# Hash products of a head in four column groups, masks placed by way of a DRAM scratch, high parts in three transfers

## The chip, the core and the metric

The kernel runs on one core of a Trainium2 chip. The metric is the device time of an execution in microseconds, less is better. The engines are named as in the profile: PE (TensorE's products), PEld (its weight loads), DVE (VectorE), ACT (ScalarE), POOL (GpSimd) and SP (SyncE, which here only issues transfers). SPq is SP's queue of issues.

## The reference

Three stages in a row. The change lies in the first.

```
# stage 1: attention within hash buckets; 2 x 8 heads, 768 tokens, head_dim 64, proj (64, 6)
q_bucket = sum(((q @ proj) > 0) * 2**bit);  k_bucket likewise
scores = where(q_bucket == k_bucket, (q @ k.T) / 8, -1e9)
x = softmax(scores) @ v
# stage 2: MLP 512 -> 2048 -> 512 with g = P(h) / Q(h), h = x @ w_in
# stage 3: mixture of 8 experts, each token to the one of its largest gate logit
```

## The kernel before

Head m = 2 i + par has pair i and parity par; most tiles exist twice, one for each parity. A head is worked in six steps c of 128 queries, each against all 768 keys. Every engine runs its own written-out order (`step(i, c)`), a loop over the pairs, and semaphores tie the engines together.

A head's q and k (64 + 64 columns) are loaded side by side (`load_qk`), transposed by PE in two halves into the bank ps_p (`turn_qk`, L459) and copied by ACT to qkT, 128 rows of 768 tokens: q in rows 0 to 63, k in rows 64 to 127 (`copy_qk`, L790). POOL makes the high parts qkT_hi (L1347) and the low parts. SP carries the high parts to their places by four SBUF to SBUF transfers (`place_hi`, L291): to k_mask, q_mask, k_cross and q_cross.

The hash bits come from `hash_qk` (L466): hash_w, 128 x 64, times the two halves of qkT. The first half of the tokens goes to rows 0 to 63 of ps_p, the second to rows 64 to 127. Each group of 64 rows holds 12 rows for q from its row 0 on and 12 for k from its row 32 on. DVE compares them with thresholds in one operation over 128 x 384 (`mask_rows`, L1014), into mask_st, and SP carries 12 rows at a time to rows 64 to 75 of q_mask and k_mask (`place_masks`, L297, four transfers a head). A score product over those 76 rows then holds the dot product and a large negative number where the buckets differ (L481); a second product adds the low parts (L483).

ps_p is shared: `turn_qk` of the next head waits for `masked`, and `hash_qk` for the copies. Within PE's step order, `turn_qk` first half stands at the start of a head, its second half in step 3, `hash_qk` at the end of step 4, and the first score product of the next head in step 4 too. That product waits for `mask_in` and `hi_in`. DVE's `mask_rows` stands at the end of step 5, behind the copy of turned probabilities (L1045).

SP's order for head m: masks of head m+1; the row inverses of head m-1 to a DRAM scratch (L309); v of head m+1 (L282); the inverses back as scale_row (L314), behind a wait for their landing; a piece of w_in (L285); q and k of head m+4, behind PE's second half of transposes (L278, L279); x of head m-2 to xT (L305); the high parts of head m+2. All waits there are on one line, L261 (`hold`). Four heads have less: the first has no masks or inverses to move in the loop, and the last four no q and k to load.

The first head does without transfers: ACT copies its high parts (L832) and DVE writes its masks straight from ps_p (`mask_first`, L1004).

Of the kernel before, what the change touches and what calls it, by code (L numbers as in the profile page):

```python
# [16 lines left out]
ALU = mybir.AluOpType  # L17
ACT = mybir.ActivationFunctionType
AX = mybir.AxisListType
F32 = mybir.dt.float32  # L20
# [3 lines left out]
P = 128  # L24

def fused_kernel(nc, q, k, v, proj, w_in, w_out, mlp_a, mlp_b, w_gate, w_ogate, w1, w2, out):
# [25 lines left out]
    ZK = 32  # L53
    HC = 64
    PAD = 8
    assert MAX_SLOTS % 2 == 1 and FE == 2 * 512 and 2 * D == P and S % (2 * P) == 0 and CD * 2 == NH and GN == HALF and KR <= P and MR <= ZK

    inv_dram = nc.dram_tensor("row_inverse_scratch", (2, S), F32).ap()
    x2_dram = nc.dram_tensor("mlp_out_scratch", (TOK, DM), F32).ap()

    with ExitStack() as ctx:
# [22 lines left out]
        with ExitStack() as stage_ab:  # L84
# [4 lines left out]
            with ExitStack() as stage_a:  # L89
                sb = sbuf(stage_a)  # L90
                q_mask = [sb(f"q_mask{i}", [P, S], F32R) for i in range(2)]
                k_mask = [sb(f"k_mask{i}", [P, S], F32R) for i in range(2)]
                q_cross = [sb(f"q_cross{i}", [P, S], F32R) for i in range(2)]
# [4 lines left out]
                k_cross = [sb(f"k_cross{i}", [P, S], F32R) for i in range(2)]  # L98
                v_raw = [sb(f"v_raw{i}", [P, QT, D]) for i in range(2)]
# [8 lines left out]
                hash_w = sb("hash_w", [P, HC])  # L108
                hash_thr = sb("hash_thr", [P, 4])
                iota_p = sb("iota_p", [P, 1])  # L110
# [20 lines left out]
        with ExitStack() as stage_c:  # L131
# [64 lines left out]

        (ident_made, iota_made, zero_made, consts_in, ab_in, hash_made, coef_ps, coef_made, abs_made) = map(sem, (
            "ident_made", "iota_made", "zero_made", "consts_in", "ab_in", "hash_made", "coef_ps", "coef_made", "abs_made"))
        qk_in = [sem(f"qk_in{i}") for i in range(2)]
# [73 lines left out]
        def _(sp):  # L273
# [25 lines left out]

# [27 lines left out]
            place_hi(1)  # L327
            sp.wait_ge(masked, 2)
            place_masks(1)
            load_v(1, 1)  # L330
# [117 lines left out]
        def _(pe):  # L448
# [13 lines left out]
            def hash_qk(i, par):  # L462

                pe.wait_ge(qk_copied, 4 * i + 2 * par + 2)
                for hb in range(2):
                    mm = pe.matmul(ps_p[HC * hb:HC * (hb + 1), 0:HALF], hash_w[:],  # L466
                                   qkT[:, hb * HALF:(hb + 1) * HALF], start=True, stop=True)
                mm.then_inc(hashed, 1)

            def scores(i, c, first=False):  # L470

                par, j, slot = c // QT, c % QT, c % 2
                if j == 0:
                    pe.wait_ge(mask_in[par], 64 * (i + 1))
                    pe.wait_ge(hi_in[par], 64 * (i + 1))
                    pe.wait_ge(qk_parts, 4 * i + 2 * par + 2)
# [76 lines left out]
            keep_clock(2)  # L553
            pe.wait_ge(hash_made, 6)
            hash_qk(0, 0)
# [3 lines left out]
            pe.wait_ge(zero_made, 3)  # L559
# [4 lines left out]
            scores(0, 1, first=True)  # L564
            pe.wait_ge(masked, 1)
            hash_qk(0, 1)
# [211 lines left out]
        def _(act):  # L778
# [51 lines left out]
            for target, rows, part in ((k_mask, slice(0, D), slice(D, P)), (k_cross, slice(0, D), slice(D, P)),  # L830
                                       (q_mask, slice(0, D), slice(0, D)), (q_cross, slice(D, P), slice(0, D))):
                act.activation(target[0][rows, :], qkT_hi[part, :], ACT.Copy).then_inc(hi_in[0], 16)  # L832
            act.wait_ge(qk_parts, 2)
# [157 lines left out]
        def _(dve):  # L991
# [5 lines left out]
            def mask_first():  # L997

                dve.wait_ge(hashed, 1)
                for hb in range(2):  # L1000
                    cols = slice(hb * HALF, (hb + 1) * HALF)
                    for target, row in ((k_mask, HC * hb + ZK), (q_mask, HC * hb)):
                        rows = slice(row, row + MR)
                        dve.tensor_scalar(target[0][D:KR, cols], ps_p[rows, 0:HALF], hash_thr[rows, 2:3],  # L1004
                                          hash_thr[rows, 3:4], ALU.is_ge, ALU.mult).then_inc(mask_in[0], 16)
                dve.wait_ge(mask_in[0], 64)
# [41 lines left out]
            def step(i, c):  # L1048
# [8 lines left out]
                if c % QT == 5 and there(i + 1, 0):  # L1057
# [6 lines left out]
            dve.memset(hash_w[:], 0.0).then_inc(zero_made, 1)  # L1064
            dve.memset(hash_thr[:], 0.0).then_inc(zero_made, 1)
            dve.wait_ge(zero_made, 3)
            dve.wait_ge(iota_made, 1)
            dve.tensor_scalar(hash_thr[:, 0:1], iota_p[:], float(BITS), TINY, ALU.is_lt, ALU.mult).then_inc(abs_made, 1)
            dve.tensor_scalar(hash_thr[:, 1:2], iota_p[:], float(ZK + BITS), TINY,
                              ALU.is_ge, ALU.mult).then_inc(abs_made, 1)  # L1070
            dve.wait_ge(abs_made, 2)
            dve.tensor_tensor(hash_thr[0:HC, 2:3], hash_thr[0:HC, 0:1], hash_thr[0:HC, 1:2],
                              ALU.add).then_inc(hash_made, 1)
            for hb in range(2):
                dve.memset(hash_thr[HC * hb:HC * hb + ZK, 3:4], 1.0).then_inc(abs_made, 1)
                dve.memset(hash_thr[HC * hb + ZK:HC * (hb + 1), 3:4], -BIG).then_inc(abs_made, 1)
            dve.wait_ge(hash_made, 1)
            dve.tensor_copy(hash_thr[HC:P, 2:3], hash_thr[0:HC, 2:3]).then_inc(hash_made, 1)
            dve.wait_ge(consts_in, 32)
            dve.tensor_copy(hash_w[0:D, 0:BITS], proj2[0:D, :]).then_inc(hash_made, 1)  # L1080
            dve.tensor_scalar(hash_w[0:D, BITS:MR], proj2[0:D, :], -1.0, None, ALU.mult).then_inc(hash_made, 1)
            dve.tensor_scalar(hash_w[D:P, ZK:ZK + BITS], proj2[D:P, :], -1.0, None, ALU.mult).then_inc(hash_made, 1)
            dve.tensor_copy(hash_w[D:P, ZK + BITS:ZK + MR], proj2[D:P, :]).then_inc(hash_made, 1)
            dve.wait_ge(abs_made, 6)
            dve.wait_ge(hash_made, 6)
            hi_of_first()
# [254 lines left out]
        def _(pool):  # L1341
            def hi_of_qk(i, par):

                pool.wait_ge(qk_copied, 4 * i + 2 * par + 2)
                if 2 * i + par > 0:
                    pool.wait_ge(hi_in[1 - par], 64 * (i + par))
                pool.tensor_scalar(qkT_hi[:], qkT[:], 1.0, 0.0, ALU.mult, ALU.add).then_inc(qk_hi_made, 1)  # L1347
# [207 lines left out]
```

## Time and profile before

| | |
|---|---|
| median of 3 runs | 822.98 us (821.36 to 823.01) |
| the profiled execution | 822.91 us |
| its span, first to last instruction | 820.9 us |
| PE busy | 785.3 us (96%) |
| DVE, ACT, POOL busy | 81%, 72%, 42% |
| granted clock of TensorE, mean | 0.986 of full |

The profile is of one execution. A line such as L466 is a line of the kernel's file. Busy time does not count waits, semaphores or the issuing of transfers. The attention stage ends near 258 us; the other stages follow.

### The profile page before, as it was taken

What the parts mean: (1) busy time and instruction counts of PE and PEld (TensorE: products, weight loads), DVE (VectorE), ACT (ScalarE), POOL (GpSimd) and SP (SyncE); (2) the same over time, 40 slices, a digit from 0 to 9 for tenths busy, and PEclk for the clock granted to TensorE, in tenths of its full rate; (3) what the DMA queues carried; (4) which work ended last, traced back from release to release, by engine and by line L of the source; (5) the groups of instructions that cost most, each with busy time, mean ns of one, the idle gap of its engine ahead of it and who ended that gap; (6) DMA issues with size and microseconds to landing.
All of it is one profiled execution on the core that took longest, in us unless ns stands there. A gap on an engine that the chain in (4) does not pass through costs nothing.

```text
span 820.9 us, 16572 instructions
## 1 busy us (share of the span) xinstructions
PE 785.3 (96%) x5050; PEld 678.1 (83%) x5050; DVE 662.0 (81%) x1101; ACT 589.6 (72%) x1046; POOL 347.6 (42%) x319
## 2 busy tenths in 40 slices
PE   8999999999998799999999999996999999999995
PEld 6888888888887688999899999976788888888884
DVE  5777777777785899788877878767899999999982
ACT  5666766767666688776676777642799988988973
POOL 5365565564643213222222222211356765565452
PEclk9999999999999999999999999997899999999999
DMA  5666786786644320100010010044782113516930
GB/s 128 141 149 159 164 180 145 174 179 146 157 98 117 109 77 2 39 1 0 0 38 0 0 38 0 1 142 165 273 288 80 38 51 111 170 45 213 373 124 1
DMA packets 75236, 88.64 MB, mean 108 GB/s; under 512 B 34355, under 2 KB 51459, under 8 KB 75204
## 3 DMA queue, kind: packets, MB, share of 16 engines
q1 hardware_dynamic: 72004, 80.11, 35.6%
q0 software_dynamic: 3040, 8.13, 3.0%
q8 instruction: 17, 0.28, 0.1%
q14 instruction: 15, 0.12, 0.1%
q10 hardware_dynamic: 160, 0.00, 0.0%
HBM read 108.82 MB, written 8.18 MB: 143 GB/s over the span
## 4 chain that ended last, share of the span: by engine, by line
PE 85%; DVE 7%; ACT 2%; issue 2%; DMA 2%; POOL 1%; DVEq 0%; SPq 0%; POOLq 0%; ACTq 0%
PE ps_s L583 14%; PE ps_t L751 13%; PE ps_s L728 13%; PE ps_t L601 9%; PE ps_o L510 9%; PE ps_t L496 7%; PE ps_o L601 4%; PE ps_s L481 4%; PE ps_s L483 3%; PE ps_s L737 2%; PE ps_p L459 2%; PE ps_p L466 1%; DVE mask_st L1014 1%; PE ps_o L715 1%; PE ps_p L642 1%
## 5 line engine op out<-in xcount | busy, mean ns | idle before, releaser
L1460 POOL TENSOR_TENSOR g_lo<-num_b,g_hi 128x384 fp32r<-128x384 f32 x64 | 65.8, 1028 | 217.3 <-ACT g_hi L875 128.1
L583 PE MATMUL ps_s<-xT,win_hi 128*128 (+1 forms) x512 | 133.0, 340 | 0.0
L1019 DVE TENSOR_REDUCE row_max<-ps_s 128x1 f32<-128x768 f32 x96 | 91.0, 948 | 44.9 <-PE ps_s L483 44.8
L1296 DVE TENSOR_TENSOR w_lo<-w_raw,w_hi 128x1024 fp32r<-128x1024 f32 x76 | 124.9, 1701 | 2.3 <-ACT w_hi L930 0.6
L795 ACT ACTIVATE probs<-ps_s,exp_bias,exp_scale 128x768 f32<-128x768 f32 x96 | 95.4, 993 | 9.1 <-DVE exp_bias L1031 8.9
L583 PEld LDWEIGHTS ps_s<-xT,win_hi 128*128 128x128 f32 x512 | 92.7, 189 | 3.8 <-issue 0.3
L801 ACT ACTIVATE probsT<-ps_t 128x384 f32<-128x384 f32 x96 | 47.3, 492 | 60.4 <-PE ps_t L496 60.4
L583 PE MATMUL ps_s<-xT,win_lo 128*128 (+1 forms) x256 | 86.2, 337 | 0.0
L496 PE MATMUL ps_t<-ident,probs 128*128 128x128 f32 x576 | 80.3, 276 | 0.9 <-DVE probsT L1045 0.9
L510 PE MATMUL ps_o<-probsT,v_raw 128*64 128x128 f32 x1152 | 76.3, 277 | 1.9 <-DVE probsT L1045 1.9
L930 ACT ACTIVATE w_hi<-w_raw 128x1024 fp32r<-128x1024 f32 x76 | 76.5, 1062 | 0.8 <-DMA w_raw<-in_moe_w_dram 0.6
L510 PEld LDWEIGHTS ps_o<-probsT,v_raw 128*64 128x64 f32 x1152 | 62.8, 137 | 16.9 <-issue 12.0
L938 ACT ACTIVATE w_hi<-w_raw 128x1024 fp32r<-128x1024 f32 x76 | 75.0, 1062 | 1.7 <-DMA w_raw<-in_moe_w_dram 1.6
L481 PE MATMUL ps_s<-k_mask,q_mask 76*128 76x384 f32 x192 | 73.8, 384 | 1.4 <-ACT qkT L790 0.9
L496 PEld LDWEIGHTS ps_t<-ident,probs 128*128 128x128 f32 x576 | 65.3, 140 | 8.1 <-issue 4.1
L1304 DVE TENSOR_TENSOR w_lo<-w_raw,w_hi 128x1024 fp32r<-128x1024 f32 x57 | 66.2, 1212 | 5.6 <-ACT w_hi L938 5.4
L1123 DVE SCALAR_TENSOR_TENSOR num_b<-num_b,coef,den_b 128x384 f32<-128x384 f32 x64 | 40.2, 629 | 32.9 <-ACT den_b L865 31.2
L483 PE MATMUL ps_s<-k_cross,q_cross 128*128 128x384 f32 x192 | 65.3, 340 | 0.0
L728 PE MATMUL ps_s<-w_hi,xgT_hi 128*128 128x512 f32 x152 | 61.7, 406 | 1.7 <-DVE xgT_lo L1309 1.7
L751 PE MATMUL ps_t<-w_hi,hT_hi 128*128 128x512 f32 x152 | 60.7, 399 | 1.2 <-issue 1.2
L1045 DVE COPY probsT<-ps_t 128x384 f32<-128x384 f32 x96 | 52.9, 551 | 9.9 <-PE ps_t L496 8.5
L728 PE MATMUL ps_s<-w_hi,xgT_lo 128*128 128x512 f32 x152 | 60.0, 395 | 0.0
(210 smaller groups left out, 1959.6 us busy)
## 6 DMA issues: line engine op xcount, KB each, us to landing
w_raw<-in_moe_w_dram SPq DMA_DIRECT2D x152, 512.0 KB
xT<-x_st SPq DMA_DIRECT2D x32, 192.0 KB, 3.7
scale_row<-row_inverse_scratch SPq DMA_DIRECT2D x32, 191.8 KB, 3.7
win_raw<-in_moe_w_in_dram SPq DMA_DIRECT2D x16, 256.0 KB, 3.9
x_sb<-in_moe_w_out_dram SPq DMA_DIRECT2D x16, 256.0 KB, 2.8
qk_raw<-in_q_dram SPq DMA_DIRECT2D x16, 192.0 KB, 3.2
qk_raw<-in_k_dram SPq DMA_DIRECT2D x16, 192.0 KB, 3.8
v_raw<-in_v_dram SPq DMA_DIRECT2D x16, 192.0 KB, 3.3
```

What stands on the lines that cost most here:

```text
L481: pe.matmul(ps_s[slot][:, hb, 0:HALF], q_mask[par][0:KR, j * P:(j + 1) * P], k_mask[par][0:KR, cols], start=True, stop=False)
L483: mm = pe.matmul(ps_s[slot][:, hb, 0:HALF], q_cross[par][:, j * P:(j + 1) * P], k_cross[par][:, cols], start=False, stop=True)
L496: mm = pe.transpose(ps_t[hb][:, t * P:(t + 1) * P], probs[c % 2][:, col:col + P], ident[:])
L510: mm = pe.matmul(ps_o[g * D:(g + 1) * D, b * P:(b + 1) * P], v_raw[par][:, t, :], probsT[(QT * par + 2 * b + g) % 4][:, t, :], start=(t == ...
L583: mm = pe.matmul(h_bank[f % 4], a[w], xT[:, c, blocks, l, :], start=(c == 0 and n == 0), stop=(c == CD - 1 and n == 2))
L601: mm = pe.matmul(acc_bank[m][:], a[:, rows], b[:, f, :], start=(f == 0 and n == 0), stop=(f == NF - 1 and n == 2))
L728: mm = pe.matmul(h_slot[b], x[:, c, :], w[par][:, c, cols], start=(c == 0 and n == 0), stop=(c == CD - 1 and n == 2))
L751: mm = pe.matmul(y_ps[:], a[:, f, :], b[:, f, :], start=(f == 0 and n == 0), stop=(f == NE - 1 and n == 2))
L795: act.activation(probs[c % 2][:].rearrange("p (b n) -> p b n", b=2), ps_s[c % 2][:, :, 0:HALF], ACT.Exp, bias=exp_bias[:, c:c + 1], scale= ...
L930: act.activation(w1_hi[par][:, c, :], w1_raw[:, c, :], ACT.Copy).then_inc(w1_hi_made, 1)
L1019: dve.tensor_reduce(row_max[:, c:c + 1], ps_s[c % 2][:, :, 0:HALF], AX.XY, ALU.max).then_inc(maxed, 1)
L1296: dve.tensor_tensor(w1_lo[par][:, c, :], w1_raw[:, c, :], w1_hi[par][:, c, :].bitcast(F32), ALU.subtract).then_inc(w1_lo_made, 1)
```

## The change

The hash products are four of a quarter of the tokens each (192), in four groups of 32 rows of ps_p; hash_w is 128 x 32, with q's 12 rows from row 0 and k's 12 from row 12. The mask operation covers 128 x 192. Its result goes by one transfer to a DRAM scratch; SP waits until it has landed and reads it back with two transfers, one for q_mask and one for k_mask, 12 rows of four pieces. k_mask and k_cross become the two planes of one tile, so that one transfer from a source read twice fills both; place_hi has three transfers. The first head keeps the old form, with tables of its own (first_w, first_thr), and DVE makes the new tables beside the old.

```diff
-                k_mask = [sb(f"k_mask{i}", [P, S], F32R) for i in range(2)]
+                k_both = [sb(f"k_both{i}", [P, 2, S], F32R) for i in range(2)]
+                k_mask = [k_both[i][:, 0, :] for i in range(2)]
+                k_cross = [k_both[i][:, 1, :] for i in range(2)]
-                mask_st = sb("mask_st", [P, HALF])
+                mask_st = sb("mask_st", [P, QUARTER])
...
             def place_hi(par):
                 hi = qkT_hi[:].bitcast(F32)
-                for target, rows, part in ((k_mask, slice(0, D), slice(D, P)), (q_mask, slice(0, D), slice(0, D)),
-                                           (k_cross, slice(0, D), slice(D, P)), (q_cross, slice(D, P), slice(0, D))):
-                    sp.dma_start(target[par][rows, :].bitcast(F32), hi[part, :]).then_inc(hi_in[par], 16)
+                sp.dma_start(k_both[par][0:D, :, :].bitcast(F32),
+                             hi[D:P, :].unsqueeze(1).to_broadcast([D, 2, S])).then_inc(hi_in[par], 16)
+                for target, rows in ((q_mask, slice(0, D)), (q_cross, slice(D, P))):
+                    sp.dma_start(target[par][rows, :].bitcast(F32), hi[0:D, :]).then_inc(hi_in[par], 16)
+
+            def store_masks(par):
+                sp.dma_start(mask_dram[par], mask_st[:]).then_inc(mask_out, 16)
 
             def place_masks(par):
-                for hb in range(2):
-                    cols = slice(hb * HALF, (hb + 1) * HALF)
-                    for target, row in ((q_mask, HC * hb), (k_mask, HC * hb + ZK)):
-                        sp.dma_start(target[par][D:KR, cols].bitcast(F32),
-                                     mask_st[row:row + MR, :]).then_inc(mask_in[par], 16)
+                quarters = mask_dram[par].rearrange("(g r) n -> r g n", r=HQ)
+                for target, row in ((q_mask, 0), (k_mask, MR)):
+                    sp.dma_start(target[par][D:KR, :].bitcast(F32).rearrange("r (g n) -> r g n", n=QUARTER),
+                                 quarters[row:row + MR, :, :]).then_inc(mask_in[par], 16)
...
                         hold(sp, masked, m + 2)
+                        store_masks(1 - par)
+                        hold(sp, mask_out, 16 * (m + 1))
                         hold(sp, scored, QT * m)
                         place_masks(1 - par)
...
             def hash_qk(i, par):
 
                 pe.wait_ge(qk_copied, 4 * i + 2 * par + 2)
-                for hb in range(2):
-                    mm = pe.matmul(ps_p[HC * hb:HC * (hb + 1), 0:HALF], hash_w[:],
-                                   qkT[:, hb * HALF:(hb + 1) * HALF], start=True, stop=True)
+                for g in range(4):
+                    mm = pe.matmul(ps_p[HQ * g:HQ * (g + 1), 0:QUARTER], hash_w[:],
+                                   qkT[:, g * QUARTER:(g + 1) * QUARTER], start=True, stop=True)
                 mm.then_inc(hashed, 1)
...
             def mask_rows(i, par, first=False):
                 dve.wait_ge(hashed, 2 * i + par + 1)
                 if not (first and par == 0):
-                    dve.wait_ge(mask_in[1 - par], 64 * (i + par))
-                dve.tensor_scalar(mask_st[:], ps_p[:, 0:HALF], hash_thr[:, 2:3], hash_thr[:, 3:4],
+                    dve.wait_ge(mask_out, 16 * (2 * i + par - 1))
+                dve.tensor_scalar(mask_st[:], ps_p[:, 0:QUARTER], hash_thr[:, 2:3], hash_thr[:, 3:4],
                                   ALU.is_ge, ALU.mult).then_inc(masked, 1)
```

In the prologue DVE zeroes first_w and first_thr beside hash_w, makes the thresholds of the first head as before, then nine small operations for the new hash_thr (32 rows made, then copied to the other three groups), and after proj has landed four writes of first_w and four of hash_w. The counts that PE and POOL wait for follow the new numbers of transfers (48 for hi_in, 32 for mask_in, a head).

## Rows read from the trace of the kernel before

**Rows 1.** The page, chain that ended last, by engine.

```profile
PE 85%; DVE 7%; ACT 2%; issue 2%; DMA 2%; POOL 1%; DVEq 0%; SPq 0%; POOLq 0%; ACTq 0%
```

**Rows 2.** Windows: length, busy by engine (instructions), clock, DMA share, GB/s.

```profile
45.00:210.00 165.00, 162.98 (x1555) 137.99 (x1555) 123.08 (x284) 114.70 (x241) 95.96 (x87) 1.00 0.74 163
...
158.10:170.40 12.30, 12.10 (x112) 9.99 (x112) 9.08 (x21) 8.41 (x19) 8.85 (x8) 1.00 0.92 197
```

**Rows 3.** Timeline of PE, heads 2 and 10: start, length, operation, count, idle.

```profile
44.83 0.55 PE L459 MATMUL ps_p<-ident,qk_raw 128*128 128x128 f32 x3 [0.20 <-DVE mask_st L1014]
...
162.74 0.87 PE L466 MATMUL ps_p<-qkT,hash_w 128*64 128x384 f32 x4
163.44 0.82 PE L510 MATMUL ps_o<-probsT,v_raw 128*64 128x128 f32 x12
...
165.43 0.34 PE L483 MATMUL ps_s<-k_cross,q_cross 128*128 128x384 f32 x1
165.98 0.55 PE L459 MATMUL ps_p<-ident,qk_raw 128*128 128x128 f32 x3 [0.20 <-DVE mask_st L1014]
...
177.01 0.42 PE L481 MATMUL ps_s<-k_mask,q_mask 76*128 76x384 f32 x1
```

**Rows 4.** Timeline of DVE around the masks of head 11.

```profile
164.78 0.56 DVE L1045 COPY probsT<-ps_t 128x384 f32<-128x384 f32 x1 [0.46 <-PE ps_t L496]
165.25 0.67 DVE L1014 TENSOR_SCALAR mask_st<-ps_p,hash_thr 128x384 f32<-128x384 f32 x1
```

**Rows 5.** A longer DVE copy out of ps_p: count, least, median, longest ns.

```profile
L1148 DVE COPY x2T<-ps_p x3: 684/684/684, 353.0 to 371.0; 128x512 f32<-128x512 f32 x3
```

**Rows 6.** Timeline of SP's issues, heads 2 and 10, and its wait for PE.

```profile
45.03 0.82 SPq L297 DMA_DIRECT2D q_mask<-mask_st  x1
...
161.69 0.62 SPq L278 DMA_DIRECT2D qk_raw<-in_q_dram  x1
...
165.00 0.50 SPq L291 DMA_DIRECT2D k_mask<-qkT_hi  x1
...
166.91 0.62 SPq L291 DMA_DIRECT2D q_cross<-qkT_hi  x1
168.26 0.83 SPq L297 DMA_DIRECT2D q_mask<-mask_st  x1
...
170.70 0.71 SPq L297 DMA_DIRECT2D k_mask<-mask_st  x1
171.63 0.35 SPq L309 DMA_DIRECT2D row_inverse_scratch<-row_inv  x1
...
173.31 1.15 SPq L314 DMA_DIRECT2D scale_row<-row_inverse_scratch  x2
174.74 0.39 SPq L285 DMA_DIRECT2D win_raw<-in_moe_w_in_dram  x1
176.84 0.62 SPq L278 DMA_DIRECT2D qk_raw<-in_q_dram  x1
...
SPq L261 <- PE ps_p L459: 1.4, 1, 1.4
```

**Rows 7.** DMA issues (us to landing): at 166.91, 91.54 and 95.59; page.

```profile
q_cross<-qkT_hi SPq DMA_DIRECT2D x1, 192.0 KB, 4.6
...
q_cross<-qkT_hi SPq DMA_DIRECT2D x1, 192.0 KB, 5.4
row_inverse_scratch<-row_inv SPq DMA_DIRECT2D x1, 3.0 KB, 2.2
...
mlp_out_scratch<-x_sb SPq DMA_DIRECT2D x12, 256.0 KB, 2.0
```

**Rows 8.** Timeline of the start: DVE, then PE, with idle before.

```profile
4.47 0.16 DVE L1080 COPY hash_w<-proj 64x6 f32<-64x6 f32 x1 [2.16 <-DMA proj<-in_proj_dram]
7.53 0.56 DVE L995 CAST qkT_hi<-qkT 128x768 fp32r<-128x768 f32 x1 [2.54 <-ACT qkT L790]
...
16.21 0.52 PE L459 MATMUL ps_p<-ident,qk_raw 128*128 128x128 f32 x3 [0.87 <-DVE mask_st L1014]
```

More of the change, by code:

```diff
@@ L54, in fused_kernel @@
     HC = 64
+    HQ = 32
+    QUARTER = S // 4
     PAD = 8
-    assert MAX_SLOTS % 2 == 1 and FE == 2 * 512 and 2 * D == P and S % (2 * P) == 0 and CD * 2 == NH and GN == HALF and KR <= P and MR <= ZK
+    assert MAX_SLOTS % 2 == 1 and FE == 2 * 512 and 2 * D == P and S % (2 * P) == 0 and CD * 2 == NH and GN == HALF and KR <= P and 2 * MR <= HQ
     inv_dram = nc.dram_tensor("row_inverse_scratch", (2, S), F32).ap()
+    mask_dram = nc.dram_tensor("hash_mask_scratch", (2, P, S // 4), F32).ap()
     x2_dram = nc.dram_tensor("mlp_out_scratch", (TOK, DM), F32).ap()
@@ L97, in fused_kernel @@
                 row_inv = sb("row_inv", [P, STEPS])
-                k_cross = [sb(f"k_cross{i}", [P, S], F32R) for i in range(2)]
+                q_cross = [sb(f"q_cross{i}", [P, S], F32R) for i in range(2)]
                 v_raw = [sb(f"v_raw{i}", [P, QT, D]) for i in range(2)]
@@ L107, in fused_kernel @@
                 proj2 = sb("proj2", [P, BITS])
-                hash_w = sb("hash_w", [P, HC])
-                hash_thr = sb("hash_thr", [P, 4])
+                hash_w = sb("hash_w", [P, HQ])
+                hash_thr = sb("hash_thr", [P, 6])
+                first_w = sb("first_w", [P, HC])
+                first_thr = sb("first_thr", [P, 4])
                 iota_p = sb("iota_p", [P, 1])
@@ L328, in _ @@
             sp.wait_ge(masked, 2)
+            store_masks(1)
+            sp.wait_ge(mask_out, 16)
             place_masks(1)
@@ L464, in hash_qk, with hash_first @@
                 pe.wait_ge(qk_copied, 4 * i + 2 * par + 2)
+                for g in range(4):
+                    mm = pe.matmul(ps_p[HQ * g:HQ * (g + 1), 0:QUARTER], hash_w[:],
+                                   qkT[:, g * QUARTER:(g + 1) * QUARTER], start=True, stop=True)
+                mm.then_inc(hashed, 1)
+            def hash_first():
+                pe.wait_ge(first_made, 6)
+                pe.wait_ge(qk_copied, 2)
                 for hb in range(2):
-                    mm = pe.matmul(ps_p[HC * hb:HC * (hb + 1), 0:HALF], hash_w[:],
+                    mm = pe.matmul(ps_p[HC * hb:HC * (hb + 1), 0:HALF], first_w[:],
                                    qkT[:, hb * HALF:(hb + 1) * HALF], start=True, stop=True)
@@ L473, in scores @@
                 if j == 0:
-                    pe.wait_ge(mask_in[par], 64 * (i + 1))
-                    pe.wait_ge(hi_in[par], 64 * (i + 1))
+                    pe.wait_ge(mask_in[par], 32 * (i + 1))
+                    pe.wait_ge(hi_in[par], 48 * (i + 1))
                     pe.wait_ge(qk_parts, 4 * i + 2 * par + 2)
@@ L564, in _ @@
             scores(0, 1, first=True)
+            pe.wait_ge(hash_made, 4)
             pe.wait_ge(masked, 1)
@@ L831, in _ @@
                                        (q_mask, slice(0, D), slice(0, D)), (q_cross, slice(D, P), slice(0, D))):
-                act.activation(target[0][rows, :], qkT_hi[part, :], ACT.Copy).then_inc(hi_in[0], 16)
+                act.activation(target[0][rows, :], qkT_hi[part, :], ACT.Copy).then_inc(hi_in[0], 12)
             act.wait_ge(qk_parts, 2)
@@ L1003, in mask_first @@
                         rows = slice(row, row + MR)
-                        dve.tensor_scalar(target[0][D:KR, cols], ps_p[rows, 0:HALF], hash_thr[rows, 2:3],
-                                          hash_thr[rows, 3:4], ALU.is_ge, ALU.mult).then_inc(mask_in[0], 16)
-                dve.wait_ge(mask_in[0], 64)
+                        dve.tensor_scalar(target[0][D:KR, cols], ps_p[rows, 0:HALF], first_thr[rows, 2:3],
+                                          first_thr[rows, 3:4], ALU.is_ge, ALU.mult).then_inc(mask_in[0], 8)
+                dve.wait_ge(mask_in[0], 32)
                 dve.sem_inc(masked, 1)
@@ L1070, in _ @@
+            dve.tensor_scalar(first_thr[:, 1:2], iota_p[:], float(ZK + BITS), TINY,
                               ALU.is_ge, ALU.mult).then_inc(abs_made, 1)
             dve.wait_ge(abs_made, 2)
-            dve.tensor_tensor(hash_thr[0:HC, 2:3], hash_thr[0:HC, 0:1], hash_thr[0:HC, 1:2],
-                              ALU.add).then_inc(hash_made, 1)
+            dve.tensor_tensor(first_thr[0:HC, 2:3], first_thr[0:HC, 0:1], first_thr[0:HC, 1:2],
+                              ALU.add).then_inc(first_made, 1)
@@ L1074, in _ @@
             for hb in range(2):
[L1075 to L1078, printed above, removed]
+                dve.memset(first_thr[HC * hb:HC * hb + ZK, 3:4], 1.0).then_inc(abs_made, 1)
+                dve.memset(first_thr[HC * hb + ZK:HC * (hb + 1), 3:4], -BIG).then_inc(abs_made, 1)
@@ new lines, in _ @@
+            dve.wait_ge(first_made, 1)
+            dve.tensor_copy(first_thr[HC:P, 2:3], first_thr[0:HC, 2:3]).then_inc(first_made, 1)
+            dve.tensor_scalar(hash_thr[0:HQ, 0:1], iota_p[0:HQ, :], float(BITS), TINY, ALU.is_lt, ALU.mult).then_inc(thr_made, 1)
+            dve.tensor_scalar(hash_thr[0:HQ, 1:2], iota_p[0:HQ, :], float(MR + BITS), TINY,
+                              ALU.is_ge, ALU.mult).then_inc(thr_made, 1)
+            dve.tensor_scalar(hash_thr[0:HQ, 4:5], iota_p[0:HQ, :], float(MR), None, ALU.is_lt).then_inc(thr_made, 1)
@@ new lines, in _ @@
+            dve.tensor_scalar(hash_thr[0:HQ, 5:6], iota_p[0:HQ, :], float(MR), -BIG, ALU.is_ge, ALU.mult).then_inc(thr_made, 1)
+            dve.wait_ge(thr_made, 4)
+            dve.tensor_tensor(hash_thr[0:HQ, 2:3], hash_thr[0:HQ, 0:1], hash_thr[0:HQ, 1:2], ALU.add).then_inc(thr_made, 1)
+            dve.tensor_tensor(hash_thr[0:HQ, 3:4], hash_thr[0:HQ, 4:5], hash_thr[0:HQ, 5:6], ALU.add).then_inc(thr_made, 1)
+            dve.wait_ge(thr_made, 6)
+            for g in range(1, 4):
+                dve.tensor_copy(hash_thr[HQ * g:HQ * (g + 1), 2:4], hash_thr[0:HQ, 2:4]).then_inc(thr_made, 1)
@@ L1079, in _ @@
             dve.wait_ge(consts_in, 32)
+            dve.tensor_copy(first_w[0:D, 0:BITS], proj2[0:D, :]).then_inc(first_made, 1)
+            dve.tensor_scalar(first_w[0:D, BITS:MR], proj2[0:D, :], -1.0, None, ALU.mult).then_inc(first_made, 1)
+            dve.tensor_scalar(first_w[D:P, ZK:ZK + BITS], proj2[D:P, :], -1.0, None, ALU.mult).then_inc(first_made, 1)
+            dve.tensor_copy(first_w[D:P, ZK + BITS:ZK + MR], proj2[D:P, :]).then_inc(first_made, 1)
             dve.tensor_copy(hash_w[0:D, 0:BITS], proj2[0:D, :]).then_inc(hash_made, 1)
@@ L1084, in _ @@
             dve.wait_ge(abs_made, 6)
-            dve.wait_ge(hash_made, 6)
+            dve.wait_ge(first_made, 6)
+            dve.wait_ge(thr_made, 9)
             hi_of_first()
```

24 lines of the change are left out of this document (11 added, 13 removed).

## The prediction

> **What bounds the kernel now.** I read the page first. The chain that ended last is TensorE work for 85% of the span [rows 1]. The change touches the attention stage only, so I asked for busy time by stage: from 45 to 210 us PE is busy 162.98 of 165.00 us, and the DMA engines carry a share of 0.74, the highest of any stage [rows 2]. The reader should keep both numbers: PE is the bound, and the transfers are not far behind. The timeline of PE in one head then shows the only gap that repeats: the transposes of the next q and k (L459) start at 165.98, 0.20 us after the last score product, begun at 165.43, has ended [rows 3]. They waited for the mask operation of VectorE, which ran from 165.25 for 0.67 [rows 4], because both use the bank ps_p. The same rows repeat each 15.15 us, once a head.
>
> Last I read SP's queue, because the change puts a wait into it. SP issues nearly without rest: from one load_qk (161.69) to the next (176.84) it waits for PE by 1.4 us only [rows 6]. The DMA engines are nearly full for 12.3 us of that head, up to the end of the high parts (share 0.92) [rows 2].
>
> **Hash products.** Before: two products of 384 tokens, as four instructions that start two by two, 0.70 us from the first to the attend product behind them [rows 3]. Two column groups do run side by side: all four, one after the other, would take twice 0.64. After: four products of 192 tokens in four groups, eight instructions. If four groups overlap as two do, two rounds of 0.16 and the 0.06 that was over now give about 0.40, a gain of 0.30. The bounds are 0.35 for a perfect half, 0.70 if only two groups run at once (no gain), and 1.28 if none overlap (0.58 worse). I take 0.40, nearest to what the two groups show. The Trainium skill ("TensorEngine Tiling (Array Packing)", Theoretical Speedup) gives up to 2x for 64 columns and up to 4x for 32; the trace agrees for 64 columns, and no row of before shows 32. Heads 2 to 15 have this in the loop: 14 x 0.30 = 4.2 us.
>
> **Mask operation.** It now covers 192 elements instead of 384. The slope comes from two copies out of PSUM, 512 elements in 684 ns and 384 in 0.56 us [rows 4, 5]: about 1 ns an element, so 0.67 becomes 0.47. The chain copy, mask, L459 ends 0.20 us sooner beside what the hash gives, and PE, which is idle for 0.20 there, can use all of it. There are 13 such waits in the loop: 2.6 us. VectorE's other work does not move: score products, not the mask, release the next row maximum.
>
> **Prologue.** VectorE makes 14 more small operations. One stands ahead of its wait of 2.16 us for proj, nine fall into that wait, and the four behind it are over long before its next work at 7.53 [rows 8]; such an operation takes 0.16 there. Without that cover they would cost about 1.5 us. The mask of head 1 comes 0.5 us sooner while PE waits 0.87 us for it [rows 8]; the exponentials follow, so I take 0.4. PE's side is then 4.2 + 2.6 + 0.4 = 7.2 us, and its own pace is 15.15 - 0.50 = 14.65 us a head.
>
> **SP's queue, step by step.** The high parts go out in three transfers for four: 2.53 us (165.00 to 167.53) becomes about 1.9. The masks were four issues, 168.26 to 171.41, 3.15 us [rows 6]. They become one store (96 KB), a wait in SP's queue for its landing, and two issues of the same kind, 1.6 us. Queued behind that wait are the store of the inverses, the load of v, the scales, w_in, the next q and k, the placing of x and the next high parts; PE waits for the masks themselves, at the first score product of the next head.
>
> The wait, L, is the unknown. A 256 KB store to DRAM lands in a median of 2.0 us when little else moves [rows 7]. Here it does not stand alone: it is issued 0.73 us behind the high parts (the gap from 167.53 to 168.26), that is 1.9 + 0.73 = 2.63 us after their first issue. The last high part landed at 166.91 + 4.6 = 171.5, 6.5 us after the first issue at 165.00; in another head that transfer took 0.8 us more, 5.4 [rows 7]. The queue keeps its order, as far as the trace shows it: in the head with 5.4 (landed at 96.94) a 3 KB store issued at 95.59 took 2.2 us and landed 0.85 behind it, while at 171.63, with the queue drained, the same store was over in less than 1.7 [rows 6, 7]. So L = 6.5 - 2.63, and 0.5 for the store's own 96 KB at 197 GB/s [rows 2]: 4.4 us. Bounds: 2.0, the plain store, and 5.2, with the slower high part. The bytes of the high parts are the same in three transfers, so that saving shortens the issue and not the drain. The Trainium skill ("DMA: Bandwidth & Descriptors", Queues, rings and completion order) says that descriptors of one queue start in order on each DMA engine; the landings agree.
>
> SP's least cycle is the sum of its pieces [rows 6]: load_qk to high parts 3.31; high parts 1.9; gap 0.73; L; two waits passed 0.2; masks 1.6; gap 0.2; inverse to scales 1.7; scales to w_in 1.43; w_in to load_qk 0.7. That is 11.8 + L. (The same pieces before: 3.31 + 2.53 + 0.73 + 3.15 + 0.2 + 1.7 + 1.43 + 0.7 = 13.75, plus the 1.4 of waiting for PE, is the head of 15.15.) With L = 4.4 the cycle is 16.2 us, 1.55 more than PE's pace of 14.65. SP would be the new bound.
>
> How long until PE feels it: PE needs the masks 11.0 us into a head (177.01 - 165.98) [rows 3]. In head 2 SP begins its masks 0.2 us into the head (45.03 against 44.83) [rows 3, 6]; after the change the store goes at 0.1, is landed at 4.5, the second mask transfer is issued at 5.5 and lands 2.2 later (the slowest of the small transfers) at 7.7: 3.3 us early. Each cycle with all its loads, for heads 3 to 12, eats 1.55 of it: 15.5 - 3.3 = 12.2 us of waits on PE. The last cycles have no load_qk and are short enough.
>
> **Sum.** The profiled execution took 822.91 us (its span 820.9 and 2.0 around it), and the median of the runs is 822.98. 822.9 - 7.2 + 12.2 = 827.9. What decides is L alone: below 3.2 there are no waits, at 3.9 waits and gains are even, and each 0.1 us more costs about 1 us.
>
> **Rivals.** (1) The masks stay hidden: L stays below 3.2, because the store overtakes the high parts or these drain sooner. For it: masks have 3.3 us of room, and DMA engines rest right behind the high parts. Against it: the in-order landings, and that SP's only slack is 1.4 us. Time: 822.9 - 7.2 = 815.7. The Trainium skill leads to this case if its formula is taken as it stands ("DMA: Bandwidth & Descriptors", Anatomy of one DMA, measured on GpSimd's path): 2.0 us and bytes over 436 GB/s, which gives an estimate of 2.2 us for the store. (2) SP binds, but L is 3.74 to 4.06: waits of 5.6 to 8.8 us against 7.2, between 821.3 and 824.5. (3) Narrow column groups do not overlap: hash 1.28 us, PE's pace 15.15 + 0.58 - 0.20 = 15.53, 14 x 0.58 = 8.1 lost for 3.0 gained: 828.0 with L under 3.7; beside L = 4.4 the waits are 6.7 - 3.3 = 3.4 more, 831.4. For it only that twice the instructions are issued; against it the pairs that start together.
>
> **Chances.** My forecast (SP's queue binds, L over 4.06) 0.50; rival 2 0.13; L below 3.74, rival 1 and the partial cases next to it, 0.32; rival 3 0.05. A measurement here tells 0.2%, 1.65 us, from no change. So faster 0.32, same 0.13, slower 0.55. The range has to reach both sides: down to rival 1, 815.5, and up to L = 5.2 (cycle 17.0, waits 23.5 - 3.3 = 20.2, so 822.9 - 7.2 + 20.2 = 835.9), 836. Within my own case it is 824.5 to 836.
>
> **What would show it.** Hash to attend 0.40 on PE; the mask operation 0.47; SP waiting for the landing of the mask store by some 4 us in each head, load_qk to load_qk 16.2 us in the middle heads, no more wait of SP for PE's transposes, and PE idle by about 1.5 us a head before the first score product (L481) with a transfer as the releaser. If instead PE's heads are 14.65 us apart with no such idle time, L was over-sized and the prediction is wrong. It is also wrong if the transfers of scales or x fall so late that POOL or ScalarE, not the masks, holds PE.

## The result, and the profile after

The changed kernel takes 832.21 us (828.71 to 832.81, 4 runs), the kernel before 823.0 us beside it. The ratio is 1.0111, with a 95% interval of 1.0086 to 1.0136: 9.2 us slower. Predicted were 827.9 us and a range of 815.5 to 836.

The profiled execution took 828.71 us, the fastest of the four, so its trace shows less than the median lost. The page, chain that ended last, by engine and by line, answers to [rows 1]:

```profile
PE 72%; DMA 9%; SPq 8%; issue 3%; DVE 3%; ACT 2%; POOL 1%; POOLq 0%; ACTq 0%; DVEq 0%
PE ps_s L605 15%; PE ps_t L773 12%; PE ps_s L750 12%; PE ps_t L623 10%; PE ps_o L623 5%; DMA hash_mask_scratch<-mask_st 5%; PE ps_o L532 4%; PE ps_t L518 3%; SPq L298 2%; PE ps_s L503 2%; PE ps_s L759 2%; PE ps_s L505 2%; DMA row_inverse_sc
```

PE held 85% of the chain before and holds 72% now. DMA and SP's issues have 9% and 8%, for 2% and 0% before, and one transfer alone, the mask store, has 5% of the span. The windows of the same stretch, beside the first line of [rows 2]:

```profile
45.00:210.00 165.00, 157.61 (x1510) 132.68 (x1507) 115.90 (x268) 108.33 (x227) 91.53 (x83) 0.97 0.78 159
```

PE is busy 157.61 of 165 us, for 162.98 before, and does fewer instructions in it. Its granted clock has a mean of 0.97.

The queue that took the place of PE is seen in the timeline of SP's issues, one cycle from load_qk to load_qk (start, length, operation, count):

```profile
151.61 0.61 SPq L284 DMA_DIRECT2D qk_raw<-in_q_dram  x1
...
155.32 0.61 SPq L295 DMA_DIRECT2D k_both<-qkT_hi  x1
155.97 0.60 SPq L298 DMA_DIRECT2D q_mask<-qkT_hi  x1
156.61 1.37 SPq L298 DMA_DIRECT2D q_cross<-qkT_hi  x1
158.11 0.72 SPq L301 DMA_DIRECT2D hash_mask_scratch<-mask_st  x1
163.00 0.33 SPq L306 DMA_DIRECT2D q_mask<-hash_mask_scratch  x1
163.38 0.36 SPq L306 DMA_DIRECT2D k_both<-hash_mask_scratch  x1
163.86 0.34 SPq L318 DMA_DIRECT2D row_inverse_scratch<-row_inv  x1
...
165.65 1.11 SPq L323 DMA_DIRECT2D scale_row<-row_inverse_scratch  x2
167.03 0.40 SPq L291 DMA_DIRECT2D win_raw<-in_moe_w_in_dram  x1
167.78 0.60 SPq L284 DMA_DIRECT2D qk_raw<-in_q_dram  x1
```

From the store at 158.11 to the first read-back at 163.00 SP issues nothing. The whole cycle is 16.17 us, where [rows 6] had 15.15 with 1.4 of it waiting for PE. Over eight cycles (load_qk at 70.72 to load_qk at 201.14) the mean is 16.30. The waits of SP from 95 to 150 us, and of PE from 150 to 200, say the same (who waits, for whom, us in total, times, longest):

```profile
SPq L267 <- DMA hash_mask_scratch<-mask_st: 15.6, 4, 4.4
SPq L267 <- DMA row_inverse_scratch<-row_inv: 1.8, 4, 0.6
```

```profile
PE ps_s L503 <- DMA k_both<-hash_mask_scratch: 4.1, 3, 2.4
```

From 60 to 200 us SP waits for no engine at all, only for two landings (34.0 us for the mask store, 5.7 us for the inverses); PE waits for SP's masks. The timeline of PE over one late head. The score product L503 has no wait in the stretch ahead of it (first lines) and one at 165.65:

```profile
152.66 0.42 PE L503 MATMUL ps_s<-k_both,q_mask 76*128 76x384 f32 x1
153.10 0.34 PE L503 MATMUL ps_s<-k_both,q_mask 76*128 76x384 f32 x1
153.61 0.55 PE L472 MATMUL ps_p<-ident,qk_raw 128*128 128x128 f32 x3
...
163.72 0.49 PE L472 MATMUL ps_p<-ident,qk_raw 128*128 128x128 f32 x3
165.65 0.43 PE L503 MATMUL ps_s<-k_both,q_mask 76*128 76x384 f32 x1 [0.78 <-DMA k_both<-hash_mask_scratch]
...
166.54 0.53 PE L479 MATMUL ps_p<-qkT,hash_w 128*32 128x192 f32 x8
167.00 0.88 PE L532 MATMUL ps_o<-probsT,v_raw 128*64 128x128 f32 x12
...
169.39 0.55 PE L472 MATMUL ps_p<-ident,qk_raw 128*128 128x128 f32 x3
```

The hash products are seen at 166.54: eight instructions, 0.46 us to the attend product, for 0.70 in [rows 3]. The transposes L472 have no idle time in front of them, so the gap that repeated before is gone. From 153.61 to 169.39 the head takes 15.78 us; where nothing waits, in heads 2 and 3 (43.49 to 58.25 to 72.98), it takes 14.75. The mask operation, all of them (least, median, longest ns), is 0.47 as reckoned:

```profile
L1036 DVE TENSOR_SCALAR mask_st<-ps_p,hash_thr x15: 468/469/472, 14.9 to 233.3; 128x192 f32<-128x192 f32 x15
```

PE's saving is real and lies in the trace; it is waited away again. PE starts on the next stage at 263.62 us, and at 255.80 before: the attention stage lost 7.8 us. The stages behind it, which the change does not touch, were 2.0 us shorter in this execution.

### The profile page after: what moved, and what is told of

Same layout as the page of the kernel before. It is cut to its first block, busy times and chain, and to the rows that moved or that the text cites. A ratio compares the mean times of both kernels' runs of the same rounds, so it can differ in the third digit from the quotient of the medians.

```text
span 826.7 us, 16696 instructions
## 1 busy us (share of the span) xinstructions
PE 787.7 (95%) x5110; PEld 679.7 (82%) x5110; DVE 662.9 (80%) x1115; ACT 589.5 (71%) x1046; POOL 346.9 (42%) x319
## 4 chain that ended last, share of the span: by engine, by line
PE 72%; DMA 9%; SPq 8%; issue 3%; DVE 3%; ACT 2%; POOL 1%; POOLq 0%; ACTq 0%; DVEq 0%
PE ps_s L605 15%; PE ps_t L773 12%; PE ps_s L750 12%; PE ps_t L623 10%; PE ps_o L623 5%; DMA hash_mask_scratch<-mask_st 5%; PE ps_o L532 4%; PE ps_t L518 3%; SPq L298 2%; PE ps_s L503 2%; PE ps_s L759 2%; PE ps_s L505 2%; DMA row_inverse_scratch<-row_inv 2%; SPq L314 2%; SPq L323 1%
## 5 line engine op out<-in xcount | busy, mean ns | idle before, releaser
L503 PE MATMUL ps_s<-k_both,q_mask 76*128 76x384 f32 x192 | 74.9, 390 | 9.2 <-DMA k_both<-hash_mask_scratch 6.3
L532 PE MATMUL ps_o<-probsT,v_raw 128*64 128x128 f32 x1152 | 78.6, 282 | 1.3 <-DVE probsT L1067 1.3
L505 PE MATMUL ps_s<-k_both,q_cross 128*128 128x384 f32 x192 | 66.1, 344 | 0.0
L750 PE MATMUL ps_s<-w_lo,xgT_hi 128*128 128x512 f32 x152 | 60.2, 396 | 0.0
```

The source lines that it names most:

```text
L503: pe.matmul(ps_s[slot][:, hb, 0:HALF], q_mask[par][0:KR, j * P:(j + 1) * P], k_mask[par][0:KR, cols], start=True, stop=False)
L505: mm = pe.matmul(ps_s[slot][:, hb, 0:HALF], q_cross[par][:, j * P:(j + 1) * P], k_cross[par][:, cols], start=False, stop=True)
L532: mm = pe.matmul(ps_o[g * D:(g + 1) * D, b * P:(b + 1) * P], v_raw[par][:, t, :], probsT[(QT * par + 2 * b + g) % 4][:, t, :], start=(t == ...
L750: mm = pe.matmul(h_slot[b], x[:, c, :], w[par][:, c, cols], start=(c == 0 and n == 0), stop=(c == CD - 1 and n == 2))
```

## The experiments

The theory: SP waits for the landing of a store that stands behind the high parts, this makes SP's cycle longer than PE's pace, and nothing else in the change costs time. The rivals after the result: the added bytes load the DMA engines; the trip through DRAM is too long wherever it starts; the narrow hash products or the double-reading transfer cost time; PE's clock, lost in its new waits, does. Each run is compared with the kernel before on its own chip; "next stage" is the first product of the MLP on PE's timeline.

| run | median us | ratio to before, 95% interval | next stage at |
|---|---|---|---|
| no wait for the landing | 816.31 | 0.9912, 0.9883 to 0.9942 | 249.81 |
| store first | 816.01 | 0.9915, 0.9891 to 0.9938 | 250.35 |
| store on ACT's queue | 816.16 | 0.9912, 0.9882 to 0.9941 | 250.39 |
| DRAM way alone | 836.17 | 1.0146, 1.0113 to 1.0179 | 271.17 |
| store first, hash in halves | 822.73 | 1.0001, 0.9986 to 1.0015 | 255.10 |
| store first, four high parts | 816.68 | 0.9935, 0.9913 to 0.9957 | 250.05 |
| three high parts alone | 822.63 | 1.0000, 0.9986 to 1.0015 | 255.60 |
| clock kept | 832.43 | 1.0124, 1.0097 to 1.0152 | 265.28 |
| wait later | 815.70 | 0.9928, 0.9911 to 0.9945 | 250.67 |

**No wait for the landing.** The transfers are all issued, but the read-back takes a plane that was stored in the prologue.

```diff
                         store_masks(1 - par)
-                        hold(sp, mask_out, 16 * (m + 1))
                         hold(sp, scored, QT * m)
                         place_masks(1 - par)
...
-                quarters = mask_dram[par].rearrange("(g r) n -> r g n", r=HQ)
+                quarters = mask_dram[2].rearrange("(g r) n -> r g n", r=HQ)
```

> The changed kernel with the same transfers, but SP does not wait for the mask store: the read-back takes a third plane of the scratch, stored once in the prologue, so every head but the first gets the masks of head 1 (that part of the computation is changed). If the wait in SP's queue is the whole loss (my account), SP's cycle falls from 16.3 us by some 4.3 to 12.0, the heads come back to PE's own pace of 14.75 us, and the time is 816 to 817.5 us. If the loss is the DMA engines' added bytes (96 KB a head) or the narrow hash products, nothing is gained by it: 829 to 832 us.

It took 816.31 us, inside the first account's 816 to 817.5. Heads are 14.75 us apart (for instance 58.16 to 72.91), and the DMA share from 45 to 210 us is the highest of all, because the same bytes go in less time:

```profile
45.00:210.00 165.00, 164.99 (x1632) 139.78 (x1629) 124.95 (x291) 117.34 (x246) 100.04 (x91) 1.00 0.82 173
```

PE is busy all the time at a DMA share of 0.82, against 0.78 in the slower kernel. So the load on the DMA engines by itself does not hold PE. The wait does. One part of the account missed: SP's cycle did not fall to 12.0 us. It is 14.78 (load_qk at 69.11 to 187.37, eight cycles), because SP now waits for the landing of the inverses instead, from 45 to 210 us:

```profile
SPq L268 <- DMA row_inverse_scratch<-row_inv: 24.2, 10, 3.2
```

That second wait, 2.4 us a head, fits into PE's pace; one of about 4 us, as in the changed kernel, does not.

**Store first.** Two lines move: the store is issued at the end of the iteration ahead, in front of the high parts.

```diff
-                        hold(sp, masked, m + 2)
-                        store_masks(1 - par)
                         hold(sp, mask_out, 16 * (m + 1))
...
                 if more:
+                    hold(sp, masked, m + 3)
+                    store_masks(par)
                     hold(sp, qk_hi_made, m + 3)
```

> The changed kernel with the mask store issued ahead of the high parts instead of behind them, the read-back where it was. My account: the store queues behind x only, 2.6 us of issues of the high parts and a gap of 0.7 cover most of its landing, a wait of 0.3 to 1.2 us is left, SP's cycle is about 12.5 to 13.5 us and PE sets the pace again: 815.5 to 818 us. If what costs is any read-back through DRAM, wherever its store stands (latency of the round trip against the need of the masks), or the load on the DMA engines: above 823 us.

It took 816.01 us, with heads of 14.75 us. The trip through DRAM is no hindrance if the queue does other work meanwhile. The landing itself did not become quick. The tile's view of DMA to landing (least, median, longest) in this kernel:

```profile
DMA to landing us min/median/max: 1.6/3.4/5.2
```

The least, 1.6 us, belongs to the stores at 29.17 and 206.20, and those at 176.71 and 191.46 took 2.4 each. In the middle heads (43.97 to 161.95) it landed after 3.3 to 5.2 us, and SP waited for it only 5.4 us in all from 60 to 200 us, four times:

```profile
SPq L267 <- DMA hash_mask_scratch<-mask_st: 5.4, 4, 1.7
```

**Store on ACT's queue.** ScalarE issues the store behind its first exponential of the head; SP waits and reads back as in the changed kernel.

```diff
-                        hold(sp, masked, m + 2)
-                        store_masks(1 - par)
...
+                if cc == 0 and there(i, c + QT) and not (isinstance(i, int) and i == 0 and par == 0):
+                    act.wait_ge(masked, 2 * i + par + 2)
+                    act.dma_start(mask_dram[1 - par], mask_st[:]).then_inc(mask_out, 16)
```

> The changed kernel with the mask store issued from ScalarE's queue at the start of the head. Same bytes at nearly the same moment, but not behind the high parts in SP's own queue. If the order within SP's queue makes the wait, the store lands in 2.0 to 2.6 us and the time is 815.5 to 819 us. If the store is slow because all 16 DMA engines are full, whatever queue it stands in, it still lands after 4 us or more and the time stays over 826 us.

Neither of my two cases came as written. The time is that of the first, 816.16 us, and the landing that of the second: I expected 2.0 to 2.6 us for a store that stands behind nothing in its own queue, and the 14 stores took 3.9 to 6.2. This kernel's store and the one of the store-first kernel are issued within 0.02 us of each other, at 161.93 and 161.95. The DMA view of these two issues (KB, us to landing), ACT's first:

```profile
hash_mask_scratch<-mask_st ACTq DMA_DIRECT2D x1, 96.0 KB, 5.3
```

```profile
hash_mask_scratch<-mask_st SPq DMA_DIRECT2D x1, 96.0 KB, 3.4
```

So a queue of its own does not make the landing quick. That the DMA engines behind both queues are full is the reading that fits, with a share of 0.93 to 1.16 in each microsecond from 162 to 167, but no run changes that load alone. Standing ahead of the high parts in SP's queue did better in this head than standing beside them in another. The Trainium skill ("DMA: Bandwidth & Descriptors", Issuing engines are not separate DMA queues) says that transfers of all issuing engines run on the same 16 DMA engines and interleave; the 5.3 us agree. What was saved here is SP's idle time: the store left when the masks were made, at the start of the head, where SP came to it up to 6.3 us later in the changed kernel (185.35 to 191.67).

**DRAM way alone.** The kernel before, with its hash and mask operation in halves and four high parts, and the masks by way of DRAM (192 KB stored).

```diff
             def place_masks(par):
-                for hb in range(2):
-                    cols = slice(hb * HALF, (hb + 1) * HALF)
-                    for target, row in ((q_mask, HC * hb), (k_mask, HC * hb + ZK)):
-                        sp.dma_start(target[par][D:KR, cols].bitcast(F32),
-                                     mask_st[row:row + MR, :]).then_inc(mask_in[par], 16)
+                halves = mask_dram[par].rearrange("(g r) n -> r g n", r=HC)
+                for target, row in ((q_mask, 0), (k_mask, ZK)):
+                    sp.dma_start(target[par][D:KR, :].bitcast(F32).rearrange("r (g n) -> r g n", n=HALF),
+                                 halves[row:row + MR, :, :]).then_inc(mask_in[par], 16)
...
                         hold(sp, masked, m + 2)
+                        store_masks(1 - par)
+                        hold(sp, mask_out, 16 * (m + 1))
```

> The kernel before with one part of the change alone: masks by way of the DRAM scratch (two halves, 192 KB stored), hash products and mask operation as before, four high part transfers. My account: SP's cycle is as in the changed kernel or up to 0.6 longer (own bytes 0.5, a fourth high part), 16.4 to 16.9 us, and since SP sets the pace the missing 0.40 us a head on PE hardly shows: 831 to 838 us. If the narrow hash products were what cost time, this one is near 823 us.

It took 836.17 us, in the range expected. The narrow hash is not in it, so it is not what cost time. SP's cycle is 16.92 us here (load_qk at 71.97 to 207.34, eight cycles), at my upper figure. From 60 to 200 us SP waits 36.4 us for the store in eight heads, 4.5 each:

```profile
SPq L263 <- DMA hash_mask_scratch<-mask_st: 36.4, 8, 5.3
```

**Store first, hash in halves.** The store-first order and three high parts, on the hash of the kernel before.

```diff
-                for g in range(4):
-                    mm = pe.matmul(ps_p[HQ * g:HQ * (g + 1), 0:QUARTER], hash_w[:],
-                                   qkT[:, g * QUARTER:(g + 1) * QUARTER], start=True, stop=True)
+                for hb in range(2):
+                    mm = pe.matmul(ps_p[HC * hb:HC * (hb + 1), 0:HALF], hash_w[:],
+                                   qkT[:, hb * HALF:(hb + 1) * HALF], start=True, stop=True)
```

> The store-first kernel with the hash products and the mask operation of the kernel before (two groups of 64 columns, 384 tokens, 192 KB stored), three high-part transfers. It prices the hash part in a kernel where PE sets the pace. Trace of the changed kernel: hash 0.46 us for 0.70, mask operation 0.47 for 0.67, heads 14.75 for 15.15. My account: the heads are 15.15 us here and the time is 822 to 824 us, 5.5 to 7 over the store-first kernel. If the gain of that kernel came from the three transfers or from freeing SP's queue, and not from the narrow hash, this one is near 816 too.

It took 822.73 us: all that the store-first kernel gains over before, some 6.5 us, is the narrow hash with its shorter mask operation. The new way of the masks is worth nothing by itself even where it costs nothing. What it is for is to place four groups with two transfers; four groups placed straight from mask_st, without the scratch, were not run.

**Store first, four high parts**, and **three high parts alone**:

```diff
-                sp.dma_start(k_both[par][0:D, :, :].bitcast(F32),
-                             hi[D:P, :].unsqueeze(1).to_broadcast([D, 2, S])).then_inc(hi_in[par], 16)
-                for target, rows in ((q_mask, slice(0, D)), (q_cross, slice(D, P))):
-                    sp.dma_start(target[par][rows, :].bitcast(F32), hi[0:D, :]).then_inc(hi_in[par], 16)
+                for target, rows, part in ((k_mask, slice(0, D), slice(D, P)), (q_mask, slice(0, D), slice(0, D)),
+                                           (k_cross, slice(0, D), slice(D, P)), (q_cross, slice(D, P), slice(0, D))):
+                    sp.dma_start(target[par][rows, :].bitcast(F32), hi[part, :]).then_inc(hi_in[par], 16)
```

The second is the same edit the other way round, on the kernel before.

> The store-first kernel with four high-part transfers for three. With three transfers the last issue is stretched to 1.4 us, so SP hardly saved any time; with four it takes about as long. My account: no change of the pace, 815.5 to 817.5 us. If the three transfers are needed to keep SP below PE's pace: over 818 us.

> The kernel before with the three high-part transfers alone. SP has slack there and the bytes are the same: 821.5 to 824 us, no change. If one transfer that reads its source twice loads the DMA engines more (its landing was 5.7 us) and delays what follows: over 825 us. If it relieves them: under 821 us.

816.68 and 822.63 us: the third part of the change does nothing to the time of either kernel. The four issues, in the store-first kernel with them, timeline of SP:

```profile
162.25 0.49 SPq L297 DMA_DIRECT2D k_both<-qkT_hi  x1
162.79 0.59 SPq L297 DMA_DIRECT2D q_mask<-qkT_hi  x1
163.43 0.59 SPq L297 DMA_DIRECT2D k_both<-qkT_hi  x1
164.06 0.60 SPq L297 DMA_DIRECT2D q_cross<-qkT_hi  x1
```

They take 2.41 us. The three of the changed kernel took 2.66 (155.32 to 157.98): the last of them is drawn out to 1.37.

The landings did change. With four high parts the store that stands first has the least, median and longest

```profile
DMA to landing us min/median/max: 1.6/2.3/3.6
```

where the store-first kernel with three had 1.6, 3.4 and 5.2, and the DMA share from 45 to 210 us is 0.74 for 0.80, at nearly the same GB/s (175 and 174). It is not the number of transfers alone: with three of them and the hash in halves the store of 192 KB landed after 1.9 to 3.7 us. These two kernels ran on another chip than the store-first one, so what makes the landing quick stays open.

**Clock kept.** The changed kernel, with four products nobody reads ahead of the first score product of each head.

```diff
+                if j == 0 and not first:
+                    for _ in range(4):
+                        pe.matmul(ps_o[:, HALF:HALF + P], ident[:], ident[:], start=True, stop=True)
                 if j == 0:
                     pe.wait_ge(mask_in[par], 32 * (i + 1))
```

> The changed kernel with four products on the unit matrix (0.86 us at the full clock) ahead of the first score product of each head, into columns that nothing reads. In the changed kernel PE idles there by up to 2.4 us, and its granted clock fell to 0.5 for some 3 us after three of these waits. If SP sets the pace, PE's own pace of 14.75 + 0.86 = 15.6 stays below SP's 16.3 and the lost clock is hidden as well: 830 to 834 us, no change. If the clock lost in the waits is a good part of the 9 us: under 829 us. If PE sets the pace: 843 us and more.

It took 832.43 us, no change, and the heads where nothing waits were 15.64 us apart (61.32 to 76.96), as 14.75 and the products make. Adding 0.89 us of work to every head of a kernel that is bound by PE would cost over 12 us. Here it costs nothing, which is the plainest sign that SP sets the pace. The clock that PE lost in the waits is hidden in the same way: its mean from 45 to 210 us is 1.00 here for 0.97 in the changed kernel, and the time is the same.

**Wait later.** The store stays behind the high parts. Only the wait and the read-back move, behind two more issues.

```diff
                         store_masks(1 - par)
-                        hold(sp, mask_out, 16 * (m + 1))
-                        hold(sp, scored, QT * m)
-                        place_masks(1 - par)
                     hold(sp, inverted, m)
                     store_inverse(1 - par)
...
                         load_v(m + 1, 1 - par)
+                        hold(sp, mask_out, 16 * (m + 1))
+                        hold(sp, scored, QT * m)
+                        place_masks(1 - par)
                     hold(sp, inv_out, 16 * m)
```

> The changed kernel with the mask store where it was, behind the high parts, and only the wait and the read-back moved two issues later, behind the store of the inverses and the load of v, in front of the wait for the inverses. Both landings then pass together. If the place of the wait is what counts, SP's cycle loses the 1.6 us or so of the second wait and about 0.7 of issues under the first: from 16.3 to about 14.2, a little under PE's 14.75, and the time is 815.5 to 819 us. If the store has to be issued earlier for any gain: over 824 us.

It took 815.70 us. The store landed no sooner (2.9 to 5.3 us, median 4.6), but SP's waits from 60 to 200 us now read:

```profile
SPq L267 <- DMA hash_mask_scratch<-mask_st: 13.6, 9, 2.1
SPq L267 <- DVE row_inv L1063: 12.0, 10, 1.7
```

That is 1.5 us a head for the store, for about 4 before, and none for the inverses' own landing, which passes in the same time. SP's cycle is 14.90 us on average (load_qk at 69.16 to 188.38, eight cycles), where I reckoned 14.2; the sum did not have the wait for the inverses to be made (DVE row_inv), which PE's own pace sets, so this does not tell how short the cycle could be. Most heads are 14.75 us apart still, three are 14.9 to 15.0.

## Why the prediction was right

The forecast was slower, by a new bound in SP's queue. Both came, and the time was inside the range, 4.3 us over the figure forecast. By its own steps:

- **Hash products.** 0.40 us was predicted, 0.46 measured; four groups overlap, nearly as two do. Rival 3 fell with that.
- **Mask operation.** 0.47 predicted, 0.47 measured.
- **PE's pace.** 14.65 predicted, 14.75 measured. PE's side was put at 7.2 us in all. The kernels in which PE sets the pace reach the next stage 5.1 to 6.0 us sooner and are 6.2 to 6.5 us faster, so this term was too large by 1 to 2 us. Of that, 14 x 0.06 = 0.8 us is the hash. The 0.4 us of the prologue can't be told: the transposes that wait there start at 15.47 to 16.01 us in the kernels with the new hash and at 15.70 to 16.39 in those with the old.
- **L.** 4.4 us predicted. The eight stores from 77.50 to 191.67 landed after 3.5 to 5.2 us, with a mean of 4.4. The order is as the prediction had it: each of the eight landed 0.1 to 0.3 us behind the last high part (at 162.81 and 162.71 in the head above). The two pieces were off and cancel in part: the high parts took 7.1 to 7.8 us from their first issue, for 6.5, and the store's own bytes added 0.1 to 0.3, for 0.5. The order within SP's queue is not the whole cause, since the ACT run shows that another queue is no quicker.
- **SP's cycle.** 16.2 predicted, 16.30 measured, partly by luck, with two wrong terms that cancel. The high parts were put at 1.9 us and took 2.66, and the two read-backs were put at 1.6 and took 0.74 (163.00 to 163.74). The first was reckoned as issues of their usual length, the second from the issues of the old masks (0.71 to 0.83 each), where those from DRAM took 0.33 and 0.36.
- **Waits.** Masks were to be 3.3 us early in head 2 and late from there on. The first head longer than 14.75 us is head 4 (72.98 to 88.13, 15.15), and the next takes 18.2. What PE loses adds up to 13.3 us (next stage at 263.62 against 250.35 in the store-first kernel), for 12.2 predicted. But not all of it is waiting, and it is not 1.5 us in each head. From 45 to 210 us PE is idle for 7.4 us, up to 2.4 at a time, and after the three longest waits it runs at the lower clock: the head from 88.13 to 106.34 is 3.46 us too long, with a wait of 1.7 in it. The prediction had no such term. It did no harm to the sum, because SP's cycle fixes the total whichever way PE spends its slack.
- **Sum.** +4.9 us predicted, +9.2 by the medians. In the profiled execution the attention stage lost 7.8 us, 2.9 more than predicted: 1.1 more is lost to SP (13.3 for 12.2), and 1.8 less is gained on PE (5.45 for 7.2, from 255.80 to 250.35 in the store-first kernel). The other 1.4 us is no term of the sum: this execution took 828.71 us where the median is 832.21, 3.5 more, and its later stages were 2.0 us shorter than in the trace of before. Why the others of the same kernel took 832.0 to 832.8 no trace here shows; their granted clock, 0.984 to 0.986, was not lower than its 0.980. That stays open.

Rival 1, masks hidden as they stood, did not come: it needed L under 3.2, and the least in the changed kernel was 3.4. A store that stands ahead of four high parts gets there (median 2.3). Rival 2 needed an L of 3.74 to 4.06; some stores had that, the mean of 4.4 did not. The time of rival 1 was right, though: 815.7 predicted for a kernel in which PE sets the pace, and four kernels that hide the wait took 815.7 to 816.7.

The change as a whole is one good part, the narrow hash with its shorter mask operation, spoilt by the place of one wait. The store-first and wait-later kernels beat both kernels, by 0.7 to 0.9% against before.

## What to carry to other kernels

Before a wait is put into a queue that issues nearly without rest, add up the queue's least cycle and hold it against the pace of the engine it serves; here 1.4 us of rest faced a wait of 4.4. A store that is read back belongs as early in the queue as its data allow, and its wait as late as its reader allows: one of the two was enough. And do not price a landing by its size: the same 96 KB took 1.6 us and 5.2 us in one kernel, and 192 KB took 1.9 to 3.7 in another. Price it by what is issued around it.

## What the runs showed of the hardware that was not expected

**A store on another engine's queue landed no sooner while the DMA engines were nearly full**: 3.9 to 6.2 us from ACT, 3.3 to 5.2 from SP in the middle heads of the store-first kernel.

**One transfer that reads its source twice saves no time of the issuing queue.** Three issues took 2.66 us with the last drawn out to 1.37, four took 2.41. The last of three took about 1.3 us or more in every kernel that has them (all heads but one), the last of four 0.6 to 0.85.

**The read-backs from DRAM were mostly issued in half the time of the transfers from SBUF**: 0.71 to 0.83 us for 12 rows from SBUF before, mostly 0.32 to 0.36 for 12 rows of four pieces from the scratch in the changed kernel (one took 1.46; up to 0.93 in the store-first kernel). Source and shape differ both, so which of them counts is not shown.

**A short idle time halves PE's clock for a while.** The windows of the changed kernel around one late head (length, busy by engine, clock, DMA share, GB/s):

```profile
98.00:100.00 2.00, 1.40 (x12) 1.13 (x10) 1.47 (x4) 1.38 (x5) 1.08 (x2) 1.00 0.11 28
100.00:102.00 2.00, 0.89 (x4) 0.86 (x4) 0.32 (x1) 0.97 (x2) 1.92 (x2) 0.87 0.41 28
102.00:104.00 2.00, 2.00 (x18) 1.00 (x18) 1.33 (x3) 0.00 (x0) 1.83 (x3) 0.50 0.86 245
104.00:106.00 2.00, 2.00 (x17) 1.67 (x14) 0.66 (x2) 0.33 (x1) 0.35 (x1) 0.78 0.91 195
```

